# Pads that place TensorE's large operands on multiples of 1024 bytes, and three turned fold buffers in place of four

## The chip, the core and the metric

The kernel runs on one core of one Trainium2 chip. The metric is the time on the device in microseconds. Three runs of the kernel before took 651.29, 652.09 and 653.58 us, so the median is 652.09 us.

## What is computed

Three layers follow one another. The first is a linear attention with decay over 4 batches, 8 heads, 768 steps and 48 dimensions per head. The second is a layer of 8 experts, of which each token takes one, and which tokens with a non-positive skip score leave out. The third is a gated layer whose output goes through two matrices.

```python
for t in range(S):                                     # attention, S = 768
    cur = einsum('bhd,bhe->bhde', u * k[t], v[t])
    y[t] = einsum('bhd,bhde->bhe', r[t], state + cur)
    state = w * state + einsum('bhd,bhe->bhde', k[t], v[t])
x = y as (3072, 384)
e_idx = argmax(x @ w_gate)                             # experts, E = 8, F = 1024
h = maximum(x[mask] @ w1[e], 0.0)
x[mask] += gate[mask] * (h @ w2[e])
a, b = x @ w1, x @ w2                                  # gated layer, d_ff = 1024
out = (a * b @ w3) @ w_out
```

## The kernel before

Tokens are 3072 rows of 384 float32 numbers. They lie in `xbuf` in HBM between the three layers.

**Attention** (`attention`) works on tiles of 64 steps by all heads, in a software pipeline over all engines.

**Fold.** The last two matrices of the third layer are multiplied once, `wf = w3 @ w_out`, so that each token needs one product in place of two. The class `Fold` does this in 8 steps. `load` brings 128 rows of `w3` into one of two buffers `w3_in`. `turn` transposes them on TensorE into two PSUM banks (L68). `turned` copies the banks to a buffer `w3T` on ScalarE (L76); there are four of these buffers, and it waits until product i-4 has freed its buffer. `product` multiplies `w3T` by `wo` (L88, 8 float32 matmuls with 384 columns). `taken` copies the result to `wf` (L96). The steps are spread over the other work by hand. In TensorE's program of `routing` the order is: product 0 (first half), turn 1, counts of the routing, product 0 (second half), product 1, turn 2, the token lists, turn 3, product 2, turn 4, product 3, more lists, turn 5, product 4, turn 6, product 5 (first half), turn 7, product 5 (second half). Product 6 follows the experts, product 7 stands at the start of the gated layers.

**Routing** (`routing`) finds each token's expert and slot. **Experts** (`experts`): for each of 8 experts up to 224 tokens are gathered, transposed and multiplied. Float32 values are split in a high and a low part of type float32r (fp32r), and each product is the sum of three: high by high, high by low, low by high. The hidden layer (L1183) has 24 groups of three matmuls per expert, with 224 columns; the weight tiles `w1_hi` and `w1_lo` are the stationary operand. The outputs (L1197) have 2 x 8 groups of three with 384 columns of `w2_hi` or `w2_lo` as the moving operand; `h_hi` and `h_lo` are the stationary one. `Over` blocks follow only when an expert has more tokens than fit.

**Gated layers** (`gated_layers`): 6 blocks of 512 tokens. For each of 8 parts f of the 1024 columns, L1408 makes 18 matmuls of 512 columns (2 matrices x 3 parts k of the contraction x 3 products); the stationary operand is a 128 by 128 tile of `wm_hi` or `wm_lo`, the moving one `xT_hi` or `xT_lo`. ScalarE copies the first result (`a_sb`, L1465), VectorE multiplies it by the second (`g_sb`, L1488), ScalarE and VectorE split the product (`g_hi` L1468, `g_lo` L1490). L1423 then makes 12 matmuls of 384 columns (4 groups i of 128 tokens x 3 products), with `g_hi` or `g_lo` as the stationary operand and row f of `wf_hi` or `wf_lo` as the moving one. The matmuls of L1423 for part f come behind those of L1408 for part f+1.

**Where tiles lie.** The program allocates SBUF tiles in order, one behind the other, each rounded up to 32 bytes. In front of the first tile lie 16512 bytes of a partition (128 modulo 1024). `program` allocates `ident` (512 bytes), then `Fold`'s tiles (two `w3_in` and four `w3T` of 4096 bytes each, `wo` and `wf` of 12288 each), `lg` and small tables (1280 bytes together with their rounding), `wm_hi` and `wm_lo` (24576 each), and `Tables` (2656 bytes). Behind these lie, one after another in time, the tiles of attention, those of the experts (`ew_`, then `ex_` behind 96 bytes of small tiles), and those of the gated layers (`gl_`). All sizes of large tiles are multiples of 1024 bytes. Rows inside them are 512, 1024, 1536, 2048 or 4096 bytes long.

Of the kernel before, what the change touches and what calls it, by code (L numbers as in the profile page):

```python
# [10 lines left out]
ACT = mybir.ActivationFunctionType  # L11
AX = mybir.AxisListType
P = 128


def wait(eng, s, val):

    if isinstance(val, int) and val <= 0:
        return
    eng.wait_ge(s, val)  # L20


def flat(x):
    return x.rearrange("p a b -> p (a b)")
# [6 lines left out]
        pe.transpose(bank[:, 0:P], ident[:, :], ident[:, :])  # L31


class Fold:


# [3 lines left out]
    def __init__(self, nc, sb, sem, ident, s_ident, w3, w_out):  # L40
        FM, DM = w_out.shape
        self.KF, self.DM = FM // P, DM
        self.w3, self.w_out, self.ident, self.s_ident = w3, w_out, ident, s_ident
        self.w3_in = [sb(f"w3_in{i}", [P, FM]) for i in range(2)]
        self.w3T = [sb(f"w3T{i}", [P, self.KF, P]) for i in range(4)]
        self.wo = sb("wo", [P, self.KF, DM])
        self.wf = sb("wf", [P, self.KF, DM])
        self.s_w3 = [sem(f"fold_w3{i}") for i in range(2)]
        self.s_wo = [sem(f"fold_wo{i}") for i in range(2)]
        self.s_T, self.s_Tout = sem("fold_T"), sem("fold_Tout")  # L50
        self.s_W, self.s_Wout = sem("fold_W"), sem("fold_Wout")
# [19 lines left out]
    def turned(self, act, i, banks):  # L71

        wait(act, self.s_T, i + 1)
        wait(act, self.s_W, i - 3)
        for h in range(2):
            act.activation(flat(self.w3T[i % 4][:, 4 * h:4 * h + 4, :]), banks[h][:, :], ACT.Copy).then_inc(self.s_Tout, 1)  # L76

    def product(self, pe, i, bank, quarters=(0, 1, 2, 3)):

        if 0 in quarters:  # L80
            wait(pe, self.s_Tout, 2 * i + 2)
            wait(pe, self.s_Wout, i)
        n = self.KF // 4
        for q in quarters:
            for g in range(q * n, (q + 1) * n):
                if i == 0 and g % (self.KF // 2) == 0:
                    pe.wait_ge(self.s_wo[g // (self.KF // 2)], 16)
                m = pe.matmul(bank[:, 0:self.DM], self.w3T[i % 4][:, g, :], self.wo[:, g, :],  # L88
                              start=(g == 0), stop=(g == self.KF - 1), skip_group_check=True)
        if 3 in quarters:  # L90
            m.then_inc(self.s_W, 1)
# [847 lines left out]
class ExpertInputs:  # L939
# [9 lines left out]
    def __init__(self, sb, sem, w1, w2):  # L949
        E, DM, FM = w1.shape  # L950
        KD, KF = DM // P, FM // P
        self.w1, self.w2, self.NG = w1, w2, KF // 2
        self.w1_in, self.w2_in = sb("w1_in", [P, KD, FM]), sb("w2_in", [P, KF, DM])
        self.w1_hi, self.w1_lo = sb("w1_hi", [P, KD, FM], F32R), sb("w1_lo", [P, KD, FM], F32R)
        self.w2_hi, self.w2_lo = sb("w2_hi", [P, KF, DM], F32R), sb("w2_lo", [P, KF, DM], F32R)
        self.x_in = [sb(f"x_in{i}", [P, 2, DM]) for i in range(2)]
        self.token = sb("token", [P, 2], I32)
        self.gate = [sb(f"gate{i}", [P, 2]) for i in range(2)]
        self.s_x = [sem(f"x{i}") for i in range(2)]
        self.s_tok, self.s_gate, self.s_go = sem("tok"), sem("gate"), sem("go")  # L960
        self.s_w1in, self.s_w2in = sem("w1in"), sem("w2in")
        self.s_w1hi, self.s_w1lo = sem("w1hi"), sem("w1lo")
        self.s_w2hi, self.s_w2lo = sem("w2hi"), sem("w2lo")
# [541 lines left out]
def program(nc, r, k, v, w, u, moe_w_skip, moe_w_gate, moe_w1, moe_w2, moe2_w1, moe2_w2, moe2_w3, moe2_w_out, out):  # L1505
    B, H, S, D = r.shape
    N, DM = B * S, H * D
    E = moe_w_gate.shape[1]
    FM = moe2_w_out.shape[0]
    CAP = 2 * P  # L1510
    ROOM = ExpertInputs.ROOM
    NO = max(j + (N - j * (ROOM + 1)) // CAP for j in range(1, E + 1))
    NSL = (E + NO) * CAP // P
    xbuf = nc.dram_tensor("xbuf", [N, DM], F32, kind="Internal").ap()
    KD = DM // P
    with ExitStack() as c:
        def scope(ctx, prefix=""):
            def sb(n, s, d=F32):
                return ctx.enter_context(nc.sbuf_tensor(prefix + n, s, d))

            def sem(n):
                return ctx.enter_context(nc.semaphore(prefix + n))
            return sb, sem
        sb, sem = scope(c)
        s_iota = sem("s_iota")
        ident = sb("ident", [P, P])
        env = {
            "ident": ident, "s_iota": s_iota, "n_logits": E + 1,
            "w_gate": moe_w_gate, "w_skip": moe_w_skip, "wm": (moe2_w1, moe2_w2),
            "fold": Fold(nc, sb, sem, ident, s_iota, moe2_w3, moe2_w_out),  # L1530
            "s_wmlo": sem("s_wmlo"), "lg": sb("lg", [P, E + 1, N // P]), "seq": S,
            "slot_token": sb("slot_token", [P, NSL], I32),
            "slot_gate": sb("slot_gate", [P, NSL]),
            "n_over": sb("n_over", [P, 1], I32),
            "over_expert": sb("over_expert", [P, NO], I32),

            "s_scattered": [sem(f"s_scattered{i}") for i in range(2)], "n_scattered": E // 2,
            "wm_hi": sb("wm_hi", [P, 2 * KD, FM], F32R),
            "wm_lo": sb("wm_lo", [P, 2 * KD, FM], F32R),
        }  # L1540
        env["tables"] = Tables(*scope(c, "tb_"), N // P, E, NSL, CAP, ROOM, NO, S)
        attention(nc, env, r, k, v, w, u, xbuf)
        with ExitStack() as ce:
            env["experts"] = ExpertInputs(*scope(ce, "ew_"), moe_w1, moe_w2)
            routing(nc, env, N // P, E, NSL, CAP, ROOM, xbuf)
            experts(nc, env, moe_w1, moe_w2, xbuf)
        gated_layers(nc, env, xbuf, out)
# [22 lines left out]
```

## Time and profile before

| what | value |
|---|---|
| median of 3 runs | 652.09 us |
| profiled execution | 654.34 us |
| its span | 652.5 us |
| TensorE (PE) busy | 618.4 us, 95% |
| VectorE (DVE) busy | 295.1 us |
| ScalarE (ACT) busy | 215.1 us |
| mean granted clock of TensorE | 0.979 of 2.4 GHz |

The span runs from the first to the last instruction that the profiler saw; the profiled execution's own time holds 1.8 us more. Attention fills the span to about 127 us, routing to about 178 us, the experts to about 326 us, the gated layers the rest. A matmul is recorded with its start and a modelled end, and two matmuls that follow one another overlap; the time that one costs is read from start to start.

### The profile page before, as it was taken

The page shows a single profiled execution, that of the slowest core. Times are in us where ns is not written, and L with a number is a line of the kernel's source. Part 1 is how long each engine was busy: PE and PEld are TensorE (multiplying, and loading weights), DVE is VectorE, ACT ScalarE, POOL GpSimd, SP SyncE. Part 2 cuts the span into 40 slices and gives each one's busy share as a digit, 9 for nine tenths or more (in the row PEclk, how much of TensorE's full clock was granted, in tenths as well). Part 3 has the DMA queues.
Part 4 walks back from the last instruction along what each step waited for, and adds up shares of the span by engine and source line. Part 5 has one row for each costly group of instructions (what it writes and reads, how often), then busy time and mean ns, then how long its engine had stood idle before and what let it go on. Part 6 is the DMA issues. An engine that isn't in the chain of part 4 may idle for free. (4 is left out here: it accounts for less than half of the span.)

```text
span 652.5 us, 17487 instructions
## 1 busy us (share of the span) xinstructions
PE 618.4 (95%) x7391; PEld 543.1 (83%) x7391; DVE 295.1 (45%) x456; ACT 215.1 (33%) x383; POOL 149.1 (23%) x183
## 2 busy tenths in 40 slices
PE   7698989789999999999989999999999999999997
PEld 7697989646699899899958888888888888888886
DVE  5476868367077666777412232132214123223222
ACT  2144445323256554554232232132213113123112
POOL 6566767324014444333121000000000000000000
PEclk9798989879999999999999999999999999999999
DMA  9779999573165577764040002003003001001001
GB/s 128 118 140 179 192 181 215 168 278 116 32 206 214 219 262 258 254 227 150 20 151 1 1 5 93 0 1 97 1 1 97 0 1 49 1 1 48 1 1 48
DMA packets 103801, 67.77 MB, mean 104 GB/s; under 512 B 79252, under 2 KB 97816, under 8 KB 103760
## 3 DMA queue, kind: packets, MB, share of 16 engines
q1 hardware_dynamic: 75824, 57.88, 32.6%
q10 hardware_dynamic: 26144, 4.74, 4.9%
q0 software_dynamic: 1792, 4.58, 2.0%
q8 instruction: 29, 0.48, 0.3%
q14 instruction: 12, 0.10, 0.1%
HBM read 55.92 MB, written 12.19 MB: 104 GB/s over the span
## 5 line engine op out<-in xcount | busy, mean ns | idle before, releaser
L1488 DVE TENSOR_TENSOR gl_g_sb<-gl_a_sb,gl_pab 128x512 f32<-128x512 f32 x48 | 33.0, 688 | 191.0 <-ACT gl_a_sb L1465 191.0
L1408 PE MATMUL gl_pab<-gl_xT_hi,wm_lo 128*128 128x512 f32 x288 | 114.8, 398 | 0.0
L1408 PE MATMUL gl_pab<-gl_xT_lo,wm_hi 128*128 128x512 f32 x288 | 113.6, 394 | 0.0
L1408 PE MATMUL gl_pab<-gl_xT_hi,wm_hi 128*128 128x512 f32 x288 | 113.5, 394 | 0.0
L1465 ACT ACTIVATE gl_a_sb<-gl_pab 128x512 f32<-128x512 f32 x48 | 28.7, 597 | 189.2 <-PE gl_pab L1408 189.2
L1423 PE MATMUL gl_po<-gl_wf_hi,gl_g_hi 128*128 128x384 f32 x192 | 65.7, 342 | 0.7 <-DVE gl_g_lo L1490 0.7
L1423 PE MATMUL gl_po<-gl_wf_lo,gl_g_hi 128*128 128x384 f32 x192 | 64.7, 337 | 0.0
L1408 PEld LDWEIGHTS gl_pab<-gl_xT_hi,wm_lo 128*128 128x128 f32 x288 | 54.1, 188 | 12.7
L1423 PE MATMUL gl_po<-gl_wf_hi,gl_g_lo 128*128 128x384 f32 x192 | 64.5, 336 | 0.0
L1408 PEld LDWEIGHTS gl_pab<-gl_xT_lo,wm_hi 128*128 128x128 f32 x288 | 54.1, 188 | 12.1
L1408 PEld LDWEIGHTS gl_pab<-gl_xT_hi,wm_hi 128*128 128x128 f32 x288 | 54.1, 188 | 11.1
L1268 DVE TENSOR_TENSOR ew_w_lo<-ew_w_in,ew_w_hi 128x768 fp32r<-128x768 f32 x32 | 45.6, 1426 | 19.3 <-ACT ew_w_hi L1233 18.6
L1183 PE MATMUL ex_ph<-ex_xT_hi,ew_w_hi 128*128 128x224 f32 x192 | 52.8, 275 | 0.0
L1183 PE MATMUL ex_ph<-ex_xT_lo,ew_w_hi 128*128 128x224 f32 x192 | 52.8, 275 | 0.0
L1183 PE MATMUL ex_ph<-ex_xT_hi,ew_w_lo 128*128 128x224 f32 x192 | 52.7, 275 | 0.0
L1490 DVE TENSOR_TENSOR gl_g_lo<-gl_g_sb,gl_g_hi 128x512 fp32r<-128x512 f32 x48 | 33.7, 703 | 33.6 <-ACT gl_g_hi L1468 33.6
L1197 PE MATMUL ex_py<-ew_w_hi,ex_h_hi 128*96 128x384 f32 (+1 forms) x128 | 45.5, 355 | 2.1 <-DVE ex_h_lo L1272 0.9
L1197 PE MATMUL ex_py<-ew_w_lo,ex_h_hi 128*96 128x384 f32 (+1 forms) x128 | 43.2, 338 | 0.0
L1197 PE MATMUL ex_py<-ew_w_hi,ex_h_lo 128*96 128x384 f32 (+1 forms) x128 | 43.2, 337 | 0.0
L1468 ACT ACTIVATE gl_g_hi<-gl_g_sb 128x512 fp32r<-128x512 f32 x48 | 30.4, 633 | 36.2 <-DVE gl_g_sb L1488 36.2
L983 POOL DMA_INDIRECT ew_x_in<-xbuf,slot_token x16 | 18.1, 1133 | 88.8 <-DVE ex_x_new L1295 66.0
L1423 PEld LDWEIGHTS gl_po<-gl_wf_hi,gl_g_hi 128*128 128x128 f32 x192 | 36.1, 188 | 2.7 <-DVE gl_g_lo L1490 1.0
(197 smaller groups left out, 1148.8 us busy)
## 6 DMA issues: line engine op xcount, KB each, us to landing
ew_w_in<-in_moe_w SPq DMA_DIRECT2D x16, 1536.0 KB, 8.2
w_in<-in_moe_w SPq DMA_DIRECT2D x14, 512.0 KB, 6.3
k_in<-in_k SPq DMA_DIRECT2D x48, 96.0 KB, 4.3
v_in<-in_v ACTq DMA_DIRECT2D x48, 96.0 KB, 4.7
r_in<-in_r SPq DMA_DIRECT2D x48, 96.0 KB, 4.2
xbuf<-x_nat SPq DMA_DIRECT2D x24, 192.0 KB
gl_x_in<-xbuf SPq DMA_DIRECT2D x12, 384.0 KB, 4.5
out<-gl_o_sb SPq DMA_DIRECT2D x12, 384.0 KB, 2.5
```

Source lines behind the costliest of these rows:

```text
L983: pool.indirect_dma_start(self.x_in[slot][0:tokens.shape[0], i, :], None, xbuf[:, :], bass.IndirectOffsetOnAxis(ap=tokens, axis=0), bounds ...
L1183: m = pe.matmul(p_h[g][:, f % 2, 0:width(t)], a[:, k, cols], b[:, k, 0:width(t)], start=(k == 0 and n == 0), stop=(k == KD - 1 and n == 2))
L1197: m = pe.matmul(p_y[i][0:n_tok, 0:DM], a[:, f, cols], b[:, f, :], start=(f == 0 and n == 0), stop=(f == KF - 1 and n == 2))
L1268: dve.tensor_tensor(flat(w2_lo[:, 2 * g:2 * g + 2, :]), flat(w2_in[:, 2 * g:2 * g + 2, :]), flat(w2_hi[:, 2 * g:2 * g + 2, :]), ALU.subtra ...
L1408: m = pe.matmul(p_ab[f % 2][w][:, :], a[:, w * KD + k, cols], b[t.slot][:, k, :], start=(k == 0 and n == 0), stop=(k == KD - 1 and n == 2))
L1423: m = pe.matmul(p_o[i][:, 0:DM], a[f % 2][:, cols], b[:, f, :], start=(f == 0 and n == 0), stop=(f == KF - 1 and n == 2))
L1465: act.activation(a_sb[f % 2][:, :], p_ab[f % 2][0][:, :], ACT.Copy).then_inc(s_a, 1)
L1468: act.activation(g_hi[f % 2][:, :], g_sb[f % 2][:, :], ACT.Copy).then_inc(s_ghi, 1)
L1488: dve.tensor_tensor(g_sb[f % 2][:, :], a_sb[f % 2][:, :], p_ab[f % 2][1][:, :], ALU.mult).then_inc(s_g, 1)
L1490: dve.tensor_tensor(g_lo[f % 2][:, :], g_sb[f % 2][:, :], g_hi[f % 2][:, :], ALU.subtract).then_inc(s_glo, 1)
```

## The change

Pads are allocated, tiles that nothing reads or writes. Behind `ident` 384 bytes bring the fold's tiles to a multiple of 1024. Behind the small tables 768 bytes bring `wm_hi` and `wm_lo` there. Behind `Tables` 416 bytes bring the tiles of attention, experts and gated layers there. Behind the experts' small tiles 928 bytes bring `ex_` there. In exchange `Fold` has three buffers `w3T` in place of four, which frees 4096 bytes. `turned` waits for product i-3 in place of i-4. No instruction is added or removed.

```diff
+LINE = 1024
+FRONT = 128
+TABLE_BYTES = 2656
...
-        self.w3T = [sb(f"w3T{i}", [P, self.KF, P]) for i in range(4)]
+        self.w3T = [sb(f"w3T{i}", [P, self.KF, P]) for i in range(3)]
...
         wait(act, self.s_T, i + 1)
-        wait(act, self.s_W, i - 3)
+        wait(act, self.s_W, i - 2)
         for h in range(2):
-            act.activation(flat(self.w3T[i % 4][:, 4 * h:4 * h + 4, :]), banks[h][:, :], ACT.Copy).then_inc(self.s_Tout, 1)
+            act.activation(flat(self.w3T[i % 3][:, 4 * h:4 * h + 4, :]), banks[h][:, :], ACT.Copy).then_inc(self.s_Tout, 1)
...
-                m = pe.matmul(bank[:, 0:self.DM], self.w3T[i % 4][:, g, :], self.wo[:, g, :],
+                m = pe.matmul(bank[:, 0:self.DM], self.w3T[i % 3][:, g, :], self.wo[:, g, :],
...
         self.gate = [sb(f"gate{i}", [P, 2]) for i in range(2)]
+        sb("pad", [P, (LINE - 96) // 4])
...
         ident = sb("ident", [P, P])
+        sb("pad0", [P, (LINE - FRONT - 4 * P) // 4])
...
             "over_expert": sb("over_expert", [P, NO], I32),
 
+            "pad1": sb("pad1", [P, (2 * LINE - sum(-(-4 * n // 32) * 32 for n in ((E + 1) * N // P, NSL, NSL, 1, NO))) // 4]),
...
         env["tables"] = Tables(*scope(c, "tb_"), N // P, E, NSL, CAP, ROOM, NO, S)
+        sb("pad2", [P, (LINE - TABLE_BYTES % LINE) // 4])
```

## Rows read from the trace of the kernel before

**Rows 1.** The page: the engines' busy time in us, share of the span, instructions.
```profile
PE 618.4 (95%) x7391; PEld 543.1 (83%) x7391; DVE 295.1 (45%) x456; ACT 215.1 (33%) x383; POOL 149.1 (23%) x183
```

**Rows 2.** Windows: busy us per engine (instructions), then granted clock, DMA share, GB/s.
```profile
10.00:188.00 178.00, 155.02 (x4862) 133.36 (x4861) 106.84 (x191) 65.17 (x137) 89.09 (x110) 0.92 0.81 165
...
440.00:645.00 205.00, 205.00 (x995) 178.60 (x994) 54.61 (x83) 47.99 (x81) 0.00 (x0) 1.00 0.07 24
```

**Rows 3.** The chain that ended last: start us, us, what.
```profile
331.09 4.02 DMA gl_x_in<-xbuf
...
336.25 2.58 PE gl_po L88 x8
...
401.06 4.20 PE gl_pab L1408 x18
405.25 2.11 PE gl_po L1423 x12
```

**Rows 4.** Timeline, a group of L1408, first four and last: start us, us, instruction.
```profile
400.89 0.40 PE L1408 MATMUL gl_pab<-gl_xT_hi,wm_hi 128*128 128x512 f32 x1
401.13 0.39 PE L1408 MATMUL gl_pab<-gl_xT_lo,wm_hi 128*128 128x512 f32 x1
401.36 0.40 PE L1408 MATMUL gl_pab<-gl_xT_hi,wm_lo 128*128 128x512 f32 x1
401.60 0.39 PE L1408 MATMUL gl_pab<-gl_xT_hi,wm_hi 128*128 128x512 f32 x1
...
404.86 0.39 PE L1408 MATMUL gl_pab<-gl_xT_hi,wm_lo 128*128 128x512 f32 x1
```

**Rows 5.** Timeline, L1423: fifth and last matmul of part 0, then of part 1.
```profile
399.50 0.33 PE L1423 MATMUL gl_po<-gl_wf_lo,gl_g_hi 128*128 128x384 f32 x1
...
400.72 0.34 PE L1423 MATMUL gl_po<-gl_wf_hi,gl_g_lo 128*128 128x384 f32 x1
...
405.81 0.33 PE L1423 MATMUL gl_po<-gl_wf_lo,gl_g_hi 128*128 128x384 f32 x1
...
407.02 0.34 PE L1423 MATMUL gl_po<-gl_wf_hi,gl_g_lo 128*128 128x384 f32 x1
```

**Rows 6.** Timeline, L1183 of one expert: first and last of 72 matmuls.
```profile
233.79 0.27 PE L1183 MATMUL ex_ph<-ex_xT_hi,ew_w_hi 128*128 128x224 f32 x1
...
241.72 0.27 PE L1183 MATMUL ex_ph<-ex_xT_hi,ew_w_lo 128*128 128x224 f32 x1
```

**Rows 7.** Timeline, L1197: a load that waits, then two matmuls ten apart.
```profile
226.42 0.19 PEld L1197 LDWEIGHTS ex_py<-ew_w_hi,ex_h_hi 128*128 128x128 f32 x1 [0.41 <-DVE ex_h_lo L1272]
...
231.68 0.34 PE L1197 MATMUL ex_py<-ew_w_hi,ex_h_hi 128*96 128x384 f32 x1
...
233.44 0.34 PE L1197 MATMUL ex_py<-ew_w_lo,ex_h_hi 128*96 128x384 f32 x1
```

**Rows 8.** The chain: eight transposes between blocks of the gated layers.
```profile
488.52 0.87 PE gl_pab L1396 x8
```

**Rows 9.** Groups by line: xcount, busy us, mean ns, idle before and its releaser.
```profile
L1490 DVE TENSOR_TENSOR gl_g_lo<-gl_g_sb,gl_g_hi 128x512 fp32r<-128x512 f32 x48 | 33.7, 703 | 33.6 <-ACT gl_g_hi L1468 33.6
...
L1465 ACT ACTIVATE gl_a_sb<-gl_pab 128x512 f32<-128x512 f32 x48 | 28.7, 597 | 189.2 <-PE gl_pab L1408 189.2
...
L445 ACT ACTIVATE kT<-p_K 128x512 f32<-128x512 f32 x24 | 14.3, 597 | 23.1 <-PE p_K L269 23.0
```

**Rows 10.** The tile w3T: its copies, and what ended ACT's idle time before them.
```profile
L76 ACT ACTIVATE w3T<-ro_pT x14: 592/594/597, 139.1 to 176.2; 128x512 f32<-128x512 f32 x14
...
  PE ro_pT L68: 12.3, 7
```

**Rows 11.** DMA issues: xcount, KB each, median us from issue to landing.
```profile
ew_w_in<-in_moe_w SPq DMA_DIRECT2D x16, 1536.0 KB, 8.2
```

**Rows 12.** Timeline, transposes of two experts in a row.
```profile
193.62 0.75 PE L1169 MATMUL ex_px<-ident,ew_x_in 128*128 128x128 f32 x6
210.59 0.75 PE L1169 MATMUL ex_px<-ident,ew_x_in 128*128 128x128 f32 x6
```

## The prediction

> **What bounds the kernel now.** I read the page's first lines, then the busy time by stage, then the chain that ended last, then single TensorE records. The page: PE is busy in 618.4 of 652.5 us, every other engine under half of that [rows 1]. The stages: attention and routing (to 188 us) run at a mean granted clock of 0.92, which is both levels (1.2 and 2.4 GHz) in turn; experts and gated layers are at 1.00, so at 2.4 GHz, and in the gated layers PE has no idle time from 336 to 645 us [rows 2]. The chain there is PE alone: a group of 18 `gl_pab` matmuls (L1408) takes 4.20 us, a group of 12 `gl_po` matmuls (L1423) 2.11 us, and 48 of each follow one another, with only transposes between [rows 3]. So the end moves with the spacing of these matmuls and with little else: ACT and DVE have two operations each in a step, of 0.6 to 0.7 us [rows 9], together some 2.6 us; PE needs 6.31 us for it.
>
> What matters is start to start, not a matmul's own duration, since matmuls overlap. 4.20/18 = 233.3 ns for 512 columns. 512 columns at 2.4 GHz are 213.3 ns, so 20.0 ns are lost. The starts show how: 0.24 us after the first matmul of the group and after each third one but the last, 0.23 after the others; 6 x 0.24 + 12 x 0.23 = 4.20 [rows 4] (the first four and the last stand for 18). The 384-column matmuls stand 1.21/7 = 173 ns apart once the first four are past (160.0 at 2.4 GHz, 13 lost) [rows 5]. 20 at 512 and 13 at 384: the loss grows with the columns and not with the number of weight loads. 160.0 x 13/12 is 173.3; 213.3 x 13/12 is 231.1, and 18 of these make 4.16 us, so 0.04 us of a 4.20 group are the six longer steps, a surcharge of 6.7 ns on each. The float32 product of the fold (L88, `w3T` by `wo`, 384 columns) shows no such loss: 2.58/8 = 322.5 ns [rows 3], which is two passes of 161 ns. So at half the read rate the engine keeps its clock, and at one fp32r column per cycle it doesn't. Whether this twelfth comes from where the operands start is the whole question.
>
> **The change part by part.** Tiles stand one behind the other, rounded to 32 bytes, the first at byte 16512. Added up, the starts modulo 1024 are: fold tiles 640, `wm_hi`/`wm_lo` 896, all of `ew_` and `gl_` 480, `ex_xT` and `ex_h` 576. After the change all are 0.
>
> *Fold with three buffers.* `turned(i)` now waits for product i-3 in place of i-4. In PE's own order product i-3 stands ahead of turn i for every i from 3 to 7 (product 2 before turn 4, 3 before 5, 4 before 6), and `turned(i)` waits for turn i anyway. ACT's idle time before these copies was ended by the turn (12.3 us in 7 waits) [rows 10]. The new condition is then already met each time: 0 us. If a product did come after its turn, `turned(i)` would hold ACT's queue with `taken(i-1)` behind it, and PE's next turn, which waits for `turned`; the price would be one product, 2.58 us [rows 3]. Products 6 and 7 read slots 0 and 1 in place of 2 and 3; nothing else writes them later.
>
> *Steady rate of the fp32r matmuls.* This decides. What the trace can say of starting bytes:
> - Inside a tensor the start moves by 512 bytes from case to case. For even f the weight tile of L1408 runs from 896 to 1408 and crosses a multiple of 1024; for odd f it runs from 384 to 896 and doesn't. The chain has 36 groups by themselves and 6 pairs (parts 0 and 1, 8.39 to 8.40 us); all groups take 4.20 us, whatever f, and one stands for them [rows 3].
> - For L1423 the moving operand starts at 480 or 992 by f, and at 992 it crosses two multiples of 1024, not one. 173 ns in both [rows 5]. The weights start at 480 or 992 by i; again nothing.
> - For L1423 weights and moving operand start in the same phase, in L1408 416 or 96 bytes apart. The twelfth is lost in both.
> So crossings of 1024 cost nothing that I can find, and the distance of the two operands neither. What no row shows is an fp32r moving operand in another phase modulo 512 in a place where it would be seen: all start at 480 there. The hidden layer's starts at 64 modulo 512, but its 224 columns (93 ns) are shorter than the spacing, 7.93/71 = 111.7 ns [rows 6], which the 128-column weight loads set: a float32 transpose, with the same load and 128 columns, is spaced 0.87/8 = 109 ns [rows 8]. Bounds: nothing, or the whole loss. A whole gain is taken at the fold's 161.25 ns for 384 columns [rows 3], and at 213.3 + 1.25 = 214.6 for 512. I take nothing, because the rows where a start was in fact moved (by 512) all read the same.
>
> The Trainium skill (SBUF — State Buffer, Specifications (TRN2), the row on cachelines) gives SBUF lines of 16 bytes and wants two hits on each. Every operand here started on a multiple of 32 before the change, so by this rule all the pads do nothing; no row here shows a line's width. The same skill (TensorE: Matmul & The Clock Gate, Back-to-back issue gap) puts matmuls N/2.4 + 2.5 ns apart, 215.8 ns for 512 columns; the trace disagrees with 233.3. By it the gates would gain 864 x 17.5 ns = 15 us if the pads removed what stands between.
>
> *Other engines.* ACT copies of 128x512 out of PSUM take 594 ns into `w3T` (phase 640) [rows 10], 597 into `kT` and 597 into `gl_a_sb` (480) [rows 9]. Half a percent between two phases; the attention tiles shift too (480 to 0), and half a percent of their 178 us bounds that at -0.9 to +0.9 us. I take 0, the `gl_` row being the nearest. DVE's 128x512 ops likewise.
>
> *Transfers.* Expert weights land 8.2 us after issue [rows 11], behind 17 us of PE work per expert [rows 12]; a tenth more or less is hidden. If that cover went, each expert would wait for it. The one load on the chain is the first `gl_x_in`, 4.02 us [rows 3]; its rows start on other bytes, I bound it at -0.5 to +0.5 us and take 0.
>
> Sum: 0 + 0 + 0 + 0. The profiled execution took 654.34 us, 1.84 around its span, and stands 2.25 above the median of 652.09. Forecast: 652.1 us, and 650.5 to 653.7 for this case alone (the terms above, and the 2.3 us that three runs spread).
>
> **The rivals.**
>
> *The twelfth comes back (chance 0.24).* The phase modulo 512 matters and at 0 the operands stream at the clock. For it: the loss is exactly steady over all 48 groups, no other engine moves it, and all moving operands that lose it share one phase. Against: 512-byte shifts and crossings cost nothing. Gates: 864 x (233.3 - 214.6) = 16.2 us. `gl_po`: 576 x (173 - 161.25) = 6.8 us, the slower first four of each group staying slower. Experts' outputs: 384 matmuls, but in the first half of each expert three waits on DVE's `h_lo` (0.41 us idle before PE's load) pace PE [rows 7], so the 18 matmuls in front of them only wait longer; 8 x 30 x 12 = 2.9 us. Hidden layer: load-bound, 0 to 576 x 2.7 = 1.5 us. Together 26 us: 626 us. ACT and DVE, at 2.6 us for a step of then 5.8, don't become the bound.
>
> *Only the surcharge goes (0.13).* The 0.24 in place of 0.23 appears in L1408, where the two operands are out of phase, and not in L1423, where they agree [rows 4, 5]. Equal phases would give 48 x 0.04 = 1.9 us; the hidden layer at the transposes' 109 ns another 1.5 us; the second half of the experts' outputs, 1.76/10 = 176 ns apart [rows 7], at 173 another 0.6. Together 4 us: 648 us.
>
> *Slower: the surcharge spreads (0.18).* With weights and moving operand both at phase 0, every load and every matmul begins on the same bytes of a line, and each pair pays the 6.7 ns that now one in three of L1408 pays. Price: gates 48 x 12 x 6.7 = 3.9 us, `gl_po` 48 x 8 x 6.7 = 2.6, experts' outputs 8 x 30 x 6.7 = 1.6: 8.1 us, 660 us. For it: some pairs do pay today, and the pads make all starts alike. Against: L1423's operands agree in phase already and pay nothing after the first four. It decides from about 300 more payers (2 us) on.
>
> *The pads don't do what they say.* If the first tile stood elsewhere than at 16512, all would sit in one wrong phase; the result would be one of the cases above. I give it nothing of its own.
>
> **How the numbers follow.** No effect 0.40, the twelfth back 0.24, surcharge gone 0.13, surcharge spread 0.18, and 0.05 for shifts in attention, where the clock changes level, 0.02 of it faster and 0.03 slower, since a stall there can drop the clock. A difference of 0.3% (2 us) is about what can be told from none. Faster 0.24 + 0.13 + 0.02 = 0.39; slower 0.18 + 0.03 = 0.21; within 0.3% 0.40. The range: no effect and surcharge gone hold 0.53, so it must take in the far cases: down to 626.0, up to 660.5. Half of each far case lies beyond its own price, (0.24 + 0.18)/2 = 0.21, so about 0.2 is left out.
>
> **What the profile after would show.** The groups in the chain settle it: `gl_pab` x18 at 4.20 and `gl_po` x12 at 2.11 is no effect; 3.86 and about 1.97 the twelfth back; 4.16 and 2.11 the surcharge gone; 4.28 and 2.16 the surcharge spread. The hidden layer's spacing of 111.7 would tell the load side by itself. A wait of `w3T` copies on `ro_pW` would disprove the fold step. The forecast is wrong if the phase modulo 512, the one thing that no row varies, has a price.

## The result, and the profile after

The change makes the kernel faster: 642.66 us (median; 641.39 to 645.26) against 652.84 (651.29 to 655.09; the three executions of before and one more), a ratio of 0.985 with a 95% interval of 0.980 to 0.989, so 10 us off, where no effect was forecast. The profiled execution took 641.39 us with a span of 639.6, 12.9 less than the span of the profile before.

The page of after: span, busy time by engine, and two parts of its queue and DMA issue lists (packets, MB, share of 16 engines; then KB each and median us from issue to landing).
```profile
span 639.6 us, 17488 instructions
...
PE 608.2 (95%) x7391; PEld 539.7 (84%) x7391; DVE 294.4 (46%) x456; ACT 216.2 (34%) x383; POOL 148.1 (23%) x183
...
q1 hardware_dynamic: 75824, 57.88, 29.9%
q10 hardware_dynamic: 26144, 4.74, 3.9%
...
ew_w_in<-in_moe_w SPq DMA_DIRECT2D x16, 1536.0 KB, 7.1
w_in<-in_moe_w SPq DMA_DIRECT2D x14, 512.0 KB, 3.3
```
PE still has the same 7391 matmuls and is the bound, but 10 us less busy than in [rows 1]. The same bytes in the same packets take less of the DMA engines: before, the two queues stood at
```profile
q1 hardware_dynamic: 75824, 57.88, 32.6%
q10 hardware_dynamic: 26144, 4.74, 4.9%
...
w_in<-in_moe_w SPq DMA_DIRECT2D x14, 512.0 KB, 6.3
```
and `ew_w_in` landed after 8.2 us [rows 11], now 7.1.

The chain of after in the first gated block (start us, us, group), which answers to [rows 3]. The pads' lines shift the code: L1408 is now L1414, L1423 is L1429, L88 is L93.
```profile
322.70 3.58 DMA gl_x_in<-xbuf
...
327.41 2.58 PE gl_po L93 x8
329.99 8.20 PE gl_pab L1414 x36
338.20 2.10 PE gl_po L1429 x12
340.30 4.12 PE gl_pab L1414 x18
```
18 `gl_pab` matmuls take 4.12 us where they took 4.20; 12 `gl_po` take 2.10, as good as before (2.11); the fold's float32 product is the same 2.58. The starts inside one group of 18, which answer to [rows 4] (the first, the tenth, and the first matmul of the next group):
```profile
391.20 0.39 PE L1414 MATMUL gl_pab<-gl_xT_hi,wm_hi 128*128 128x512 f32 x1
...
393.28 0.39 PE L1414 MATMUL gl_pab<-gl_xT_hi,wm_hi 128*128 128x512 f32 x1
...
395.32 0.33 PE L1429 MATMUL gl_po<-gl_wf_hi,gl_g_hi 128*128 128x384 f32 x1
```
The first nine take 2.08 us (231 ns each), the last nine 2.04 us, 226.7 ns each. Before, all 18 stood 233.3 ns apart on average. Neither the twelfth's return (3.86 us) nor the loss of the surcharge as I priced it (4.16) is what came.

Busy time of the first 122 us, nearly all of it attention, before and after (columns as in [rows 2]: stretch, PE, PEld, DVE, ACT, POOL, granted clock, DMA share, GB/s):
```profile
0.00:122.00 122.00, 103.75 (x4416) 98.19 (x4416) 81.51 (x160) 45.66 (x100) 77.39 (x101) 0.93 1.02 173
...
0.00:122.00 122.00, 103.30 (x4520) 97.52 (x4521) 84.76 (x163) 46.37 (x102) 80.43 (x118) 0.96 0.81 174
```
At the same GB/s the DMA engines are busy for 0.81 instead of 1.02 of the time (before, they were full), and PE gets through 104 matmuls more in the same stretch.

The stages by their first and last instructions, in us, with two figures that the experiments turn on. "Piece" is the mean time of a 192-byte packet of attention's loads; "PE slow" is the time at the lower clock level; "gates" is the mean distance of `gl_pab` matmuls in ns.
```
kernel   attention routing experts between gated  span   piece ns  PE slow  gates
before     125.8    53.4    144.3   14.9   314.2  652.5    21.3     27.3    233.4
after      121.7    52.7    140.6   14.5   310.1  639.6    15.9     17.1    229.1
```
So the 12.9 us come from three places: gated layers 4.1, attention 4.1, experts 3.7, and about 1 us between them. They are more than the medians' 10.2 us, since the profiled execution of before was slower than its median and that of after was the fastest of its four. Only the first place stood among my rivals with a mechanism, and smaller than it is.

### The profile page after: what moved, and what is told of

Read it like the earlier page. It is cut to its first block and busy times, and to the rows that moved or that the text cites. A ratio compares the mean times of both kernels' runs of the same rounds, so it can differ in the third digit from the quotient of the medians.

```text
span 639.6 us, 17488 instructions
## 1 busy us (share of the span) xinstructions
PE 608.2 (95%) x7391; PEld 539.7 (84%) x7391; DVE 294.4 (46%) x456; ACT 216.2 (34%) x383; POOL 148.1 (23%) x183
## 5 line engine op out<-in xcount | busy, mean ns | idle before, releaser
L1414 PE MATMUL gl_pab<-gl_xT_hi,wm_lo 128*128 128x512 f32 x288 | 112.9, 392 | 0.0
L1414 PE MATMUL gl_pab<-gl_xT_lo,wm_hi 128*128 128x512 f32 x288 | 112.8, 392 | 0.0
L1414 PE MATMUL gl_pab<-gl_xT_hi,wm_hi 128*128 128x512 f32 x288 | 112.3, 390 | 0.0
L1429 PE MATMUL gl_po<-gl_wf_hi,gl_g_hi 128*128 128x384 f32 x192 | 65.6, 342 | 0.7 <-DVE gl_g_lo L1496 0.7
L1429 PE MATMUL gl_po<-gl_wf_hi,gl_g_lo 128*128 128x384 f32 x192 | 64.7, 337 | 0.0
L1429 PE MATMUL gl_po<-gl_wf_lo,gl_g_hi 128*128 128x384 f32 x192 | 64.5, 336 | 0.0
L1414 PEld LDWEIGHTS gl_pab<-gl_xT_hi,wm_lo 128*128 128x128 f32 x288 | 54.0, 188 | 11.4
L1414 PEld LDWEIGHTS gl_pab<-gl_xT_lo,wm_hi 128*128 128x128 f32 x288 | 54.0, 188 | 10.6
L1414 PEld LDWEIGHTS gl_pab<-gl_xT_hi,wm_hi 128*128 128x128 f32 x288 | 54.1, 188 | 10.4
L1274 DVE TENSOR_TENSOR ew_w_lo<-ew_w_in,ew_w_hi 128x768 fp32r<-128x768 f32 x32 | 42.8, 1337 | 14.1 <-ACT ew_w_hi L1239 11.7
L989 POOL DMA_INDIRECT ew_x_in<-xbuf,slot_token x16 | 18.4, 1152 | 85.7 <-DVE ex_x_new L1301 62.7
L1429 PEld LDWEIGHTS gl_po<-gl_wf_hi,gl_g_hi 128*128 128x128 f32 x192 | 36.1, 188 | 2.5 <-DVE gl_g_lo L1496 1.0
```

The costliest lines, as they stand in the source:

```text
L989: pool.indirect_dma_start(self.x_in[slot][0:tokens.shape[0], i, :], None, xbuf[:, :], bass.IndirectOffsetOnAxis(ap=tokens, axis=0), bounds ...
L1274: dve.tensor_tensor(flat(w2_lo[:, 2 * g:2 * g + 2, :]), flat(w2_in[:, 2 * g:2 * g + 2, :]), flat(w2_hi[:, 2 * g:2 * g + 2, :]), ALU.subtra ...
L1414: m = pe.matmul(p_ab[f % 2][w][:, :], a[:, w * KD + k, cols], b[t.slot][:, k, :], start=(k == 0 and n == 0), stop=(k == KD - 1 and n == 2))
L1429: m = pe.matmul(p_o[i][:, 0:DM], a[f % 2][:, cols], b[:, f, :], start=(f == 0 and n == 0), stop=(f == KF - 1 and n == 2))
```

## The experiments

Two theories stood at the start. *Distance*: PE's spacing depends on how far the starts of weights and moving operand are apart, modulo some period, and not on where they are. *Place*: it depends on where they are (multiples of 1024). For the rest of the gain the question was whether the fold, the pads in attention, or the pads from the experts on bring it.

**The fold alone** (three buffers on the kernel before, no pads):
```
-  self.w3T = [... for i in range(4)]      wait(act, self.s_W, i - 3)
+  self.w3T = [... for i in range(3)]      wait(act, self.s_W, i - 2)
```


> The kernel before with three fold buffers in place of four and no pads; all tiles keep their starts modulo 1024 (fold 640, wm 896, the rest 480). If the fold's ring is free, as predicted, the time is that of before within 0.3% and the groups stay 4.20 us (18 gates matmuls) and 2.11 us (12 output matmuls). If fewer buffers or the shift by 4096 bytes matter by themselves, it differs by 2 us or more.

Measured: 654.31 us against 653.15, ratio 1.002 (0.999 to 1.006). In after, the tile `w3T` reads (answering to [rows 10])
```profile
L81 ACT ACTIVATE w3T<-ro_pT x14: 591/594/598, 134.4 to 171.5; 128x512 f32<-128x512 f32 x14
...
  PE ro_pT L73: 11.3, 7
```
with no wait on `ro_pW`. The fold is worth nothing that shows here, and costs nothing.

**Attention's tiles alone** (the same, with one tile ahead of attention's own, so that they start at 0 modulo 1024; everything from the experts on stays at 480):
```
+  sb("pad_at", [P, (1024 - 480) // 4])
```


> e1 and one pad of 544 bytes inside attention: only attention's tiles move from 480 to 0 modulo 1024. Theory T (transfers): the 192-byte pieces of the r and v loads lie inside 256 bytes and no longer across a boundary, their packets fall from about 22 to 16 ns, attention ends about 4 us earlier and the whole kernel is 3 to 4.5 us faster than e1, with gates groups still 4.20 us. Theory C (chance): the 4 us in attention came from where the clock's drops fell, and the time is that of e1 within 0.3%.

Measured: 651.20 us, ratio 0.997 (0.994 to 0.9995), 3.1 us below the fold alone and 1.9 below the kernel before. The intervals of the two runs against before just touch (0.994 to 0.9995, and 0.999 to 1.006), so the size is uncertain. Gates as before, `344.12 4.20 PE gl_pab L1409 x18` in the chain, but the DMA queues fall; first the fold alone, then this one:
```profile
q1 hardware_dynamic: 75824, 57.88, 32.5%
q10 hardware_dynamic: 26144, 4.74, 4.8%
...
q1 hardware_dynamic: 75824, 57.88, 29.8%
q10 hardware_dynamic: 26144, 4.74, 3.9%
```
A piece of 192 bytes takes 16.1 ns in place of 21.1, and attention ends after 120.3 us instead of 125.7. Neither PE theory speaks of this: the place of attention's tiles acts through the transfers.

**The change, with attention put back to 480:**
```
+  sb("pad_at", [P, 480 // 4])       # on top of the change
```


> The changed kernel with attention's tiles alone put back to 480 modulo 1024. Theory T: packets of 192 bytes back at about 22 ns, 3 to 4.5 us slower than the changed kernel, so about 6 us faster than before; gates groups 4.12 us. Theory C: as the changed kernel, 10 us faster than before.

Measured: 647.75 us, ratio 0.992 (0.989 to 0.995), 5.4 us below the kernel before. Piece 20.9 ns, attention 124.5 us, gates `346.98 4.12 PE gl_pab L1415 x18`. So the gates' 4.12 belongs to the pads behind attention, and the piece's 16 ns to the place of attention's tiles.

**All of the change's tiles at 480 modulo 1024**, distances among them kept:
```
-  sb("pad0", [P, (LINE - FRONT - 4 * P) // 4])
+  sb("pad0", [P, (LINE - FRONT - 4 * P + 480) // 4])
```


> The changed kernel with the first pad 480 bytes longer: every tile behind ident starts at 480 modulo 1024, so the weights and the moving operands agree with each other and none is at a multiple of 1024. Theory R (relative): TensorE's reads of weights and moving operand disturb each other by their distance, gates groups 4.12 us as in the changed kernel. Theory A (absolute): a start off a multiple of 1024 costs by itself, gates groups 4.20 us. By theory T attention is as slow as before in both. Total by R and T about 4 to 8 us faster than before, by A and T that of before.

Measured: 648.95 us, ratio 0.995 (0.992 to 0.997). The chain:
```profile
344.70 2.10 PE gl_po L1429 x12
...
346.80 4.12 PE gl_pab L1414 x18
```
The gates are what they are in after, to the hundredth. *Place* is refuted for TensorE's gates; *distance* holds. The transfers, though, are as in the kernel before (21.6 ns a piece, attention 125.4 us): for them the place does count.

**Spacing by distance, alone.** A kernel that runs 20 fp32r matmuls of 512 columns from each of six starts of the moving operand with each of nine starts of the weights, and leaves out the rest.

> Computes nothing of the reference: streams of 20 fp32r matmuls with 512 columns, each with its own weight load, for 6 starts of the moving operand by 9 starts of the weights (modulo 1024), and 5 streams with 384 columns. Theory R: the spacing depends on the distance of the two starts alone, about 227 ns where they agree (0/0, 480/480), 231 or more at distances 416 and 96, the same for equal distances. Theory A: 227 only where both are at 0. If the twelfth of the kernel before and the sixteen cycles of the one after have nothing to do with starts, all streams are alike.

Measured spacing in ns (start to start of the streams; rows: start of the moving operand, columns: of the weights, bytes modulo 1024):
```
        0     32     64     96    128    192    256    384    480
0     226.7  233.2  233.2  234.1  232.5  229.2  226.7  232.7  233.5
32    233.4  226.6  233.2  233.2  234.0  233.2  233.5  234.1  228.6
64    228.9  233.5  226.7  233.2  233.2  232.5  229.2  233.5  233.2
128   232.3  233.2  229.2  233.2  226.6  233.2  232.5  226.7  234.5
256   228.6  233.2  233.2  234.1  232.5  229.2  226.7  232.7  233.5
480   233.5  233.5  234.6  232.4  233.1  233.4  233.2  233.2  227.5
```
The first two streams in the trace, by busy time (columns as above; PEld's x20 are the 20 weight loads of each stream):
```profile
23.45:28.00 4.55, 4.55 (x22) 3.75 (x20) 0.00 (x0) 0.00 (x0) 0.00 (x0) 1.00 0.00 0
28.00:32.65 4.65, 4.65 (x21) 3.75 (x20) 0.00 (x0) 0.00 (x0) 0.00 (x0) 1.00 0.02 4
```
Twenty matmuls take 4.55 us where both operands start at 0 and 4.65 where the weights start 32 bytes on. The table repeats with 256 bytes: where both starts agree modulo 256 the spacing is 226.7, where the weights start 192 bytes further on, modulo 256, it is 229, and else some 233. Two readings at equal starts come out higher, 228.6 and 227.5: in both streams the first matmuls are slower (those of 480 and 480 start 233, 236, 224, 231, 236, 228, 233 and 230 ns apart) and the rest stand at 226.7. In the kernel before, a tile of `wm` started 416 bytes behind the start of `gl_xT` or 96 in front of it, which are both 160 bytes further on modulo 256: 233.

With 384 columns the spacing is 173.3 at equal starts and 176.7 for moving at 480 with weights at 384. But moving at 0 with weights at 64 also gives 173.3, where 512 columns give 233.2. So which distances cost is not the same for every number of columns.

**The same more finely, and with other sizes:** moving operand at 0, weights further on by 4 bytes and up.

> Computes nothing of the reference: streams of 24 fp32r matmuls, moving operand at 0 modulo 1024, weights at 28 distances from 0 to 512 bytes, many of them no multiple of 32, then streams with fewer weight columns (128, 96, 64, 32) and fewer moving columns (512, 384, 256) at distances 0 and 128. Theory R (two streams that meet): the loss per matmul grows with the weight columns and not with the moving ones at distance 0 (226.7 - 213.3 = 13.3 ns for 128 columns, so about 6.7 for 64 and 3.3 for 32), and some distance may be free of it (216 ns or less). Theory M (the moving stream alone): the loss stays when the weight columns are fewer. The period of the distances is 256 bytes by the first table, so 256 and 512 read like 0.

```
bytes   0      4      8      12     16     28     32     44     60     64
ns    226.7  232.3  230.8  230.0  233.3  235.0  233.3  230.0  230.0  233.3
bytes  96    112-160  192    208    224    240    256    512
ns    233.8   233.3  228.9  231.9  233.3  226.7  226.7  226.7

equal starts, weight columns x moving columns: 128x512 226.7, 96x512 230.0, 64x512 230.0,
32x512 231.7, 128x384 173.3, 64x384 173.3, 128x256 120.0
weights 128 bytes further on:  128x512 232.8, 96x512 231.7, 64x512 229.1,
32x512 230.6, 128x384 176.5, 64x384 173.3, 128x256 118.3
```
Even 4 bytes cost. With 512 columns nothing, here or in the table above, comes under 226.6. At 2.4 GHz 512, 384 and 256 columns are 213.3, 160.0 and 106.7 ns; the readings lie 13.4, 13.3 and 13.3 above. At equal starts that is a constant of 13.3 ns for each matmul, and no twelfth of its columns. It doesn't shrink with fewer weight columns, so it isn't the length of the weight load either; what it is stays open. Nor is it a floor: 256 columns at a distance of 128 bytes take 118.3 ns, less than at equal starts, and so do 64 weight columns by 512 (229.1 against 230.0). The price of a distance is shown for 128 weight columns with 512 columns, and at some distances with 384.

**Transfers by start, alone.** Loads of 192-byte pieces and of 4096-byte rows on one queue, nothing else running.

> Computes nothing of the reference: loads of 192-byte pieces at steps of 256 bytes, into tiles that start at 0, 32, 64, 128, 224 and 480 modulo 1024, and of 4096-byte rows into tiles that start at 0, 32, 128 and 480. Theory T: pieces at 0, 32 and 64 stay inside 256 bytes and land at one rate, pieces at 128, 224 and 480 cross a boundary and land later, by about a third; the rows differ by about 1/16 between 0 and the others. Theory C: all alike.

Measured: 16.4 to 16.9 ns a piece and 7.0 to 7.7 us for a batch of eight loads, at each of the starts 0, 32, 64, 128, 224 and 480; long rows 171 to 175 ns. The start does nothing here. That left open what in the kernel makes it count.

**Two more places for attention's tiles**, 64 and 32 modulo 1024:
```
+  sb("pad_at", [P, (1024 - 480 + 64) // 4])     # and + 32
```


> As e2, but attention's tiles at 64 modulo 1024. If only the phase modulo 64 matters to the transfers, the 192-byte packets take 16 ns; if a multiple of 256 or 1024 is needed, about 22.

> As e2, but attention's tiles at 32 modulo 1024. If the phase modulo 64 is what matters (480 is 32 modulo 64), the packets take about 22 ns; if crossing a boundary of 256 does it, about 16, since a piece of 192 bytes at 32 stays inside.

Measured: 16.1 ns a piece in both, attention 122.7 and 123.8 us (one execution each, 650.08 and 651.99 us; the kernel before took 650.39 beside them, so the whole time shows no gain here). Neither 1024 nor 64 is needed. `r_in` and `v_in` hold a piece of 192 bytes in each 256. From a start of 32 or 64 modulo 256 it ends at 224 or 256, inside one block of 256 bytes; from 480, which is 224 modulo 256, it crosses into the next. That fits all seven profiles with attention's tiles at 0, 32 or 64 (15.9 to 16.1 ns) and all five at 480 (20.9 to 21.6).

For `k_in` it does not fit. Its pieces follow each other at 192 bytes, so some cross wherever the tile starts. With the tiles at 32 three of four do, just as at 480: 18,432 of the 49,152 pieces on SP's queue. Yet only 815 pieces there took over 21 ns, where the kernel before has 16,643. Crossing by itself is therefore not what costs; the starts of `r_in` and `v_in` are.

**What makes the start count.** The loads at starts 0, 32, 64 and 480, each with one other thing running.

> Computes nothing of the reference: the loads of 192-byte pieces again into tiles at 0, 32, 64 and 480, each alone and then beside one other thing: loads on ScalarE's queue, stores of 1536-byte rows from tiles in the same phase, matmuls, ScalarE, VectorE or GpSimd working on tiles in the same phase, all together. Theory Q: two queues at once make the packets of tiles at 480 longer (22 against 16 ns). Theory W: the stores from a tile at 480 do it. Theory E: an engine's work on the same phase does it. Each shows in its own case and in the last; in all other cases the packets take about 16.6 ns as when alone.

Measured, ns a piece (us a batch of eight):
```
start                         0            32           64           480
alone                      16.3 (7.2)   16.6 (7.1)   16.9 (7.1)   16.0 (7.1)
a second queue loading     17.7 (8.7)   15.8 (8.2)   15.4 (8.0)   28.5 (11.5)
stores on a second queue   15.3         15.2         15.1         20.0
PE, ACT, DVE or POOL busy  16.1 to 17.0 at every start
all of these together      16.9 (8.4)   16.0         15.6         27.7 (12.4)
```
The second queue's loads (issue to landing, median us; a, b, c, d are 0, 32, 64, 480):
```profile
alsoa_<-in_v ACTq DMA_DIRECT2D x16, 96.0 KB, 4.1
alsob_<-in_v ACTq DMA_DIRECT2D x16, 96.0 KB, 3.8
alsoc_<-in_v ACTq DMA_DIRECT2D x16, 96.0 KB, 3.7
alsod_<-in_v ACTq DMA_DIRECT2D x16, 96.0 KB, 6.1
```
It takes traffic on a second queue: beside loads a piece at 480 takes 28.5 ns for 15.4 to 17.7. Compute engines don't matter. Attention loads `k_in` and `r_in` from SP's queue and `v_in` from ACT's, and its DMA engines were full. 480 is the only crossing start that was tried with a second queue, so the runs do not tell the crossing from the start of 224 modulo 256. The Trainium skill (DMA: Bandwidth & Descriptors, How a descriptor splits into AXI transactions) has each transaction start at a multiple of 256 bytes, so that a crossing piece needs two; the runs at 32, 64 and 480 agree in the direction, but with one queue alone there is no price for it, and `k_in`'s crossing pieces pay none either.

**The change once more**, to see how much of the experts' 3.7 us stays:

> The changed kernel once more, on the chip of e8. Theory S (settled): the steps between experts repeat as in its first profile, 17.0 us three times and then 17.4 to 18.1, and attention ends near 121.7 us. Theory L (luck): where the steps go from 17.0 to 18.8 us differs from run to run, and with it 3 us of the gain in the experts. Time about 642.7 us in both.

Measured: 643.64 us against 654.76, ratio 0.983 (0.981 to 0.985); experts 142.0 us, gated 310.1, attention 123.8. Of the experts' gain 2.3 us are left here. What moves in that stage is one wait. Longest idle times of ACT by cause (us in total, times, longest), before, after, the run at 480, and this one:
```profile
ACT wm_hi L1253 <- DMA w_in<-in_moe_w: 30.1, 6, 6.1
...
ACT wm_hi L1259 <- DMA w_in<-in_moe_w: 24.7, 6, 5.4
...
ACT wm_hi L1259 <- DMA w_in<-in_moe_w: 27.8, 6, 6.0
...
ACT wm_hi L1259 <- DMA w_in<-in_moe_w: 27.6, 6, 5.8
```
SP issues the gated layers' part `w_in` behind the expert's two loads, which put 3 MB in front of it; ACT waits for it, with the split of the next expert's weights queued behind. The steps from expert to expert, from first to first matmul of the hidden layer, in us:
```
before     17.05 17.03 18.38 18.81 18.77 17.99 17.89
at 480     17.09 17.00 16.99 18.49 18.76 17.99 17.95
again      17.06 17.00 17.00 18.47 18.81 17.62 17.56
after      17.06 17.00 17.00 17.00 18.46 17.81 17.85
```
A step is 17.0 us by PE's own work; from some expert on the late load makes it 18.5 to 18.8. The pads move the point at which this begins by one or two experts, but not in every run: with attention put back to 480 the experts have the same pads and take 143.9 us, 0.4 less than before.

**Taking that wait away**, on the change and on the kernel before:
```
-  rounds(sp, whole(sp, (load_w1, 1), (load_w2, 1), (load_wm, 0)), 2, E, 0, 0)
+  rounds(sp, whole(sp, (load_wm, 0), (load_w1, 1), (load_w2, 1)), 2, E, 0, 0)
```


> The changed kernel with the load of the third layer's matrices ahead of the two loads of the next expert in SyncE's order, in place of behind them. If the late steps between experts (17.4 to 18.8 us in place of 17.0) come from ScalarE waiting up to 5.4 us for that load with the next w2 split behind it, the waits go and each of the 8 experts takes about 17.0 us: 3 to 6 us faster than the changed kernel. If they come from VectorE held by GpSimd's subtraction of the same matrices (3.7 us), nothing or less is gained, since the subtraction stays.

> The kernel before, with no pads and four fold buffers, and only the load of the third layer's matrices ahead of the next expert's loads, as in e8. Theory K (the late load alone sets the experts' steps): the experts take 137.5 to 138.5 us as in e8, so the kernel is 6 us faster than before and the pads' share in the experts is nothing by itself. Theory P (the pads matter there): the experts take 140 us or more. Gates groups 4.20 us, attention as before.

Measured: on the change 639.44 us (ratio to before 0.977, 0.975 to 0.980), on the kernel before 647.92 (0.989, 0.986 to 0.992). The experts take 137.5 us with the pads and 137.6 without them, and all steps are 17.00 to 17.04. ACT's first waits are then for PE:
```profile
ACT ex_h_hi L1233 <- PE ex_ph L1189: 21.6, 27, 1.7
ACT ew_w_hi L1239 <- PE ex_py L1203: 16.7, 6, 3.4
```
(with the pads). The pads give the experts next to nothing of their own: they only soften a wait that another order removes.

**Is a multiple of 256 enough?** The kernel before with the new load order, four fold buffers, and pads of 128, 160 and 160 bytes, which put the tiles at multiples of 256, most of them not of 1024:
```
+  sb("pad", [P, 160 // 4])    sb("pad0", [P, 128 // 4])    sb("pad2", [P, 160 // 4])
```


> As e8, but with three pads of 128, 160 and 160 bytes that bring the tiles to multiples of 256 (most of them no multiple of 1024), and the four fold buffers of the kernel before. By the tables of m1 and m4 a distance of 256 is as good as none, and by m3, e5 and e6 a transfer needs only that a piece doesn't cross 256 bytes: gates groups 4.12 us, packets of 192 bytes at 16 ns, the time of e8 within 0.3%, some 15 us under before. If 1024 matters, it falls short of e8 by 2 us or more.

Measured: 640.06 us, ratio 0.979 (0.974 to 0.984); gates `338.04 4.12 PE gl_pab L1409 x18`, piece 16.0 ns, experts 137.5 us. Its interval overlaps that of the version with 1024 and the new order (0.975 to 0.980). 448 bytes of pads and no change of the fold do in the gates and in attention what the change's pads do. The version with the load first beats the change itself: its interval lies below that of the change beside it (0.981 to 0.985). This one's interval touches that, so of it the runs show the stages, not a proven lead.

The other stages of all kernels, one profile each, as the table above:
```
kernel          attention routing experts between gated  span   piece ns  PE slow  gates
fold alone        125.7    51.8    144.5   14.6   314.2  650.8    21.1     17.1    233.5
attention at 0    120.3    54.0    144.3   14.6   314.2  647.4    16.1     10.2    233.4
attention back    124.5    52.7    143.9   15.2   310.1  646.3    20.9     20.5    229.1
all at 480        125.4    53.4    142.7   14.6   310.3  646.3    21.6     27.3    229.1
change again      123.8    53.0    142.0   14.4   310.1  643.2    16.0     17.1
load first        120.1    54.0    137.5   14.4   310.1  636.1    16.0     13.7
before, load f.   126.4    53.9    137.6   14.7   314.2  646.8    21.4     34.1    233.4
multiples of 256  121.3    53.5    137.5   15.0   310.1  637.4    16.0     13.7    229.1
```
Attention moves by some 2 us from one profile to the next; the time that PE spends at the lower clock level moves with it (10 to 34 us), and only partly with the pads. Over all profiles it takes 125.6 us on average at 480 and 122.0 at 0, 32 or 64. That is 3.6 us less, but the time at the lower clock level differs too, 25 us on average at 480 and 16 at the other places. At an equal time there, attention takes 125.7 us at 480 against 121.7 and 123.8 (17.1 us at the lower level), and 124.5 against 122.7 and 123.8 (20.5 us, the last two being the runs at 64 and 32). So at an equal time there the gain is 0.7 to 4.0 us. Whether the shorter transfers also keep the clock up, so that the rest is theirs too, isn't shown. The run that changes only attention's place puts all of it at 3.1 us.

## Why the prediction was wrong, step by step

*Fold with three buffers, 0 us.* Right: the fold alone shows no difference that its interval (0.999 to 1.006) leaves room for beyond 0.6%, and no wait on `ro_pW` appeared.

*Steady rate of the fp32r matmuls, 0 us.* Wrong by 864 x (233.4 - 229.1) = 3.7 us, and this is the step that failed first: it put the distance of the two operands at nothing. (The gated stage as a whole lost 4.1 us; a group of each kind in the chain took 4.20 + 2.11 us and now takes 4.12 + 2.10.) Two readings led to it. I took the rows in which starts move by 512 bytes as evidence that starts don't matter; the period is 256, so they could not have shown anything. And I took "the twelfth is lost in both" (in phase in L1423, out of phase in L1408) to mean that the distance of the operands costs nothing. But the loss isn't a twelfth. It is 13.3 ns whatever the columns, and 20.0 at 512 columns when out of phase. For 384 columns in phase, 13.3 happens to be one twelfth of 160.0; for 512 out of phase, 20.0 is near one twelfth of 213.3, and the rest of it I called a surcharge. Two points, one in phase and one not, can be fitted by a share of the columns as well as by a constant plus a price; I had [rows 6] for a third size but those were bound by weight loads. The correct part was the observation behind the rival "only the surcharge goes": the two groups differ in that their operands agree in phase. It had the mechanism, and the sign; its size was off, 1.9 us where 3.7 came, because only 1 in 3 matmuls was taken to pay 6.7 ns, when all paid it (in phase all 18 would be at 226.7). Its two other terms did not come: the hidden layer kept its spacing, and the experts' outputs, 96 bytes apart before, went from 174.8 to 173.4 ns at the end of their groups (without and with the pads, both with the load first), half of what it asked, and no step of the experts got shorter by more than 0.03 us. The first nine of each group after outputs still run at 231 ns rather than 226.7, which is why the gain is 0.08 us a group and not 0.12. The streams with equal starts show such slower first matmuls too, at 480 and 480 for eight of them, without any change in the number of columns. Why is open.

*Crossings of 1024 cost nothing.* Right, and more than that: the place has no effect on the gates' matmuls, as the run at 480 and the stream at 480 and 480 show.

*Hidden layer.* Its 111.7 ns [rows 6] are 111.7 after as well, as the mean of all eight experts. The rival's 1.5 us from this place didn't come. That it is bound by loads, as the step said, fits.

*Other engines, 0 (at most 0.9 us in attention).* Right for the operations: ACT's copies take 594 (`w3T`) and 598 to 599 ns after, against 594 and 597 in [rows 9, 10]. The bound was drawn around the wrong resource, though. Attention changed by 4.1 us, by the transfers that I had not read there (how much of it through the clock is open): [rows 2] show a DMA share of 0.81 over attention and routing beside 0.07 in the gated layers, and I read only PE and the clock from them. Attention by itself, asked for as a stretch of its own, would have shown 1.02.

*Transfers, 0 us, "behind 17 us of PE work per expert".* Wrong twice. In attention the DMA engines had no time to spare, so a cheaper piece counts there. In the experts the expert's own weights are indeed hidden, as I said, but `w_in`, issued behind them, wasn't: ACT waited 30.1 us for it in six waits of up to 6.1. PE's steps of 18.4 to 18.8 us were there to be read in the timeline of before; [rows 12] show one of the 17.0 ones, and I took it for all. The pads took 3.7 us there in one profile and 2.3 in another, 0.4 with attention put back to 480, and 0.1 once the load was moved. The first `gl_x_in`, bounded at 0.5 us, gained 0.44 (4.02 to 3.58).

*The rivals.* The twelfth did not come back to PE (gates 4.12, not 3.86). Nothing got slower with equal phases: "the surcharge spreads" had it the wrong way round, since with these 512 columns equal starts are what doesn't pay. The range, 626.0 to 660.5, held the time only because it reached far on both sides, which is luck; none of its cases gives these 10 us by what brought them.

The sum as it should have been, from the measured prices: gates 3.7, attention 3.1 to 3.6, experts 0.4 to 3.7, `gl_x_in` 0.4: 7.6 to 11.4 us, where 10.2 were measured. The experts' term could not have been told closer from rows of before: it is what is left of a wait whose start moves from run to run.

*Left open:* what the constant 13.3 ns of an fp32r matmul is; why a distance of 64 bytes costs with 512 columns and not with 384, and one of 128 bytes with both and not with 256; why the first eight or nine matmuls after a change of operands are slower; why the pieces at 480 cost only beside a second queue, and `k_in`'s crossing ones not at all; and at which expert the steps turn from 17.0 to 18.8.

## What to carry to other kernels

Read every stage's DMA share as carefully as its PE share: this stage, with full DMA engines, gained when its pieces got cheaper. Pieces of 192 bytes at steps of 256 belong where each stays inside one block of 256 bytes: starts of 0, 32 and 64 served equally well here. For fp32r matmuls of 128 weight columns and 512 moving ones, start both operands at the same byte modulo 256; where that is doesn't matter. And a load that is needed early goes ahead of large ones on its queue: in this kernel that alone gave 5.8 us, more than the pads gave in the gates or in attention.

Before saying that rows exclude an effect, ask which period they could have shown: starts that move by 512 bytes say nothing about anything that repeats with 256.

## What the runs showed of the hardware

- fp32r matmuls with 128 weight columns follow one another at their columns at 2.4 GHz plus 13.3 ns (226.7, 173.3, 120.0 ns for 512, 384, 256) if both operands start at the same byte modulo 256. At 512 columns four bytes off cost 5.6 ns, most other distances 6.6; 240 bytes cost nothing, and 192 bytes 2.2 to 2.5. At 384 columns 128 or 160 bytes cost some 3 ns and 64 nothing; at 256 columns 128 bytes off is 1.7 ns quicker.
- Fewer weight columns don't make it faster at equal starts: 230.0 ns with 64 or 96, 231.7 with 32.
- Pieces of 192 bytes, one in each 256, that start at 480 and so cross a multiple of 256 bytes in SBUF take 16.0 ns on a queue alone, like any other, but 28.5 when a second queue loads likewise, and 20.0 beside stores. Pieces laid one behind the other (`k_in`) cross without a price: with all of attention's tiles at 32, SP's queue takes 16.2 ns a piece.
- The Trainium skill (TensorE: Matmul & The Clock Gate, Back-to-back issue gap) would have 215.8 ns for 512 columns. The traces disagree: no fp32r stream of 512 columns here came under 226.6.
